# Second MoE of a fused attention and two-MoE kernel: fold the first weights of all eight experts while the tokens are sorted, fetch folded weights per tile, split the second weights by halves

## The reference

```python
x = attention(q, k, v)                    # 3072 tokens x 512
logits = x @ phi                          # first MoE: 8 experts x 4 slots = 32 slots
d = softmax(logits, axis=0); c = softmax(logits, axis=1)
slot_out[e] = relu((d.T @ x)[e] @ w1[e]) @ w2[e]
x = c @ slot_out                          # 3072 x 512, of rank 32
# second MoE, top-1
logits = x @ w_gate                       # 3072 x 8
idx = argmax(logits); gate_w = softmax(logits)[idx]
for e in range(8):                        # experts that have tokens
    h = relu(x[idx == e] @ w1[e])         # 512 -> 1024
    out[idx == e] = gate_w * (h @ w2[e])  # 1024 -> 512
```

## Time and profile before

| | |
|---|---|
| median of 3 runs | 518.71 us (517.88 to 519.81) |
| the profiled execution | 519.71 us, its span 518.0 us |
| mean granted TensorE clock | 0.913 of full |
| PE busy | 456.3 us (88%) |
| DVE, ACT, POOL busy | 246.5, 197.9, 202.5 us |
| moved by DMA | 89.79 MB |
| attention and first MoE | to about 272 us of the span |
| routing | about 272 to 307 us |
| second MoE's expert work | about 307 to 518 us |

### The profile page before, as it was taken

How to read it: one execution, slowest core, us unless ns; L and a number is a source line. 1 busy time by engine, 2 the same in 40 slices (tenths; PEclk the granted TensorE clock), 3 DMA queues, 4 the chain that set the end, 5 groups by cost and what they waited for, 6 DMA issues and landing times. The chain is left out here.

```text
span 518.0 us, 9323 instructions
## 1 busy us (share of the span) xinstructions
PE 456.3 (88%) x3119; PEld 377.8 (73%) x3120; DVE 246.5 (48%) x793; ACT 197.9 (38%) x399; POOL 202.5 (39%) x182
## 2 busy tenths in 40 slices
PE   7899999999999899989985055999999999999771
PEld 7699999999999877544455043888888887887451
DVE  5457777776777633641113947233332333332451
ACT  1568877877877444111000013122222122222420
POOL 2879888888886001010000001233333333333200
PEclk9879999999999989979985557999999999999976
DMA  6598898867661088499920357211111111111100
GB/s 232 211 411 331 331 381 323 340 232 262 233 237 59 4 310 341 140 387 384 407 103 1 140 189 273 82 51 38 43 51 51 51 51 51 51 51 51 44 2 5
DMA packets 27236, 89.79 MB, mean 173 GB/s; under 512 B 3344, under 2 KB 3344, under 8 KB 27200
## 3 DMA queue, kind: packets, MB, share of 16 engines
q1 hardware_dynamic: 23936, 79.70, 41.1%
q0 software_dynamic: 3264, 9.64, 5.3%
HBM read 81.46 MB, written 8.13 MB: 173 GB/s over the span
## 5 line engine op out<-in xcount | busy, mean ns | idle before, releaser
L435 ACT ACTIVATE Pb<-Pb,nm 128x256 f32<-128x256 f32 (+1 forms) x192 | 83.7, 484 | 35.4 <-DVE nm L536 35.4
L1466 DVE SCALAR_TENSOR_TENSOR hl<-Hq,hh 128x512 fp32r<-128x512 f32 x54 | 37.3, 691 | 123.5 <-ACT hh L1435 123.5
L382 PE MATMUL O<-V,PTs 128*128 128x65 f32 x704 | 91.7, 272 | 0.0
L382 PEld LDWEIGHTS O<-V,PTs 128*128 128x128 f32 x704 | 88.3, 195 | 1.0 <-issue 1.0
L536 DVE CUSTOM_DVE_ANT_0 Pb<-S,TA 128x256 f32<-128x256 f32 (+1 forms) x192 | 68.7, 396 | 37.2 <-PE S L355 35.2
L1410 PE MATMUL Yq<-w2h,hh 128*128 128x512 f32 x200 | 84.9, 425 | 0.3 <-DVE hl L1466 0.3
L1411 PE MATMUL Yq<-w2l,hh 128*128 128x512 f32 x200 | 79.6, 398 | 0.0
L1412 PE MATMUL Yq<-w2h,hl 128*128 128x512 f32 x200 | 79.4, 397 | 0.0
L1435 ACT ACTIVATE hh<-Hq 128x512 fp32r<-128x512 f32 x54 | 32.3, 598 | 115.9 <-PE Hq L1374 87.7
L313 POOL TENSOR_TENSOR kl<-k_raw,kh 128x1632 fp32r<-128x1632 f32 x15 | 55.2, 3679 | 9.9 <-ACT kh L445 9.7
L364 PE MATMUL PT<-ident,Pb 128*128 128x128 f32 x352 | 55.9, 278 | 0.9 <-ACT Pb L435 0.9
(11 more groups left out here) (222 smaller groups left out, 585.2 us busy)
## 6 DMA issues: line engine op xcount, KB each, us to landing
mem<-in_moe_w SPq DMA_DIRECT2D x14, 2048.0 KB, 11.4
k_raw<-in_k SPq DMA_DIRECT2D x16, 816.0 KB, 7.5
q_raw<-in_q SPq DMA_DIRECT2D x16, 768.0 KB, 5.6
ext<-in_moe_w SPq DMA_DIRECT2D x6, 2048.0 KB, 19.0
V<-in_v SPq DMA_DIRECT2D x16, 715.0 KB, 4.5
c_rows<-XL POOLq DMA_DIRECT2D x1, 1536.0 KB, 14.0
Cg<-c_rows,src POOLq DMA_INDIRECT x27, 2.5
out<-Ysb,dst POOLq DMA_INDIRECT x25
```

What stands on the lines that cost most here:

```text
L382: mm = pe.matmul(O[grp % 2][:, at:at + VC], PTs[:, par, (h * kbs + kb) * P:(h * kbs + kb + 1) * P], V[:, buf, h, vb, :], start=(n == 0), s ...
L435: nc.scalar.activation(Pb[:, par, h, 0:width(g)], Pb[:, par, h, 0:width(g)], ACT.Exp, bias=nm[:, par, h:h + 1], scale=-1.0).then_inc(exp_d ...
```

## The change

- `soft_moe` also transposes `Cn` to `CT` (in a free part of `mem`), on PE after the second expert's hidden products, and SP goes on after the 16 pieces with the first weights of the second MoE, experts 0 to 5, each into the slot named by `v1_slot` once that slot's piece is used.
- `routing` and `top1_moe` are one block. PE runs 16 *units* (8 experts x 2 halves) of the fold among the sorting's matmuls: two before the rank matmuls, ten before the 24 sorting matmuls, four after. In a unit, ACT does the copies, and the remainder is made on PE: a matmul with `-I` subtracts the rounded value in place, and ACT copies the result to the lower 64 rows. All folded weights stay in `Gall`. `C4` is ordered high, remainder, high, remainder to match.
- Per tile, ACT issues two DMAs that copy the half of a tile's expert from `Gall` to `Gst` inside the on-chip memory, the number of the expert being read from a table `te`.
- The second weights of the next expert are split chunk by chunk as each half of the last tile's products is done. An expert change has no fold.
- POOL gathers three tiles ahead, copies the source column before it waits for `cg_turned`, and the destination column before it waits for `y_scaled`. DVE does `low(u, 1)`, `low(u + 1, 0)` and then the scaling of tile u, which was behind both halves of `low(u + 1)` before.

The diff, cut to its core:

```diff
@@ build
+        v1_loaded = [sem(f"v1_loaded{e}") for e in range(NE)]
+def v1_slot(mem, e):
+    n = [MEMW, MEMW + 1, 0, 1, 2, 3, MEMW, MEMW + 1][e]
+    return mem[:, n, :]
@@ soft_moe, SP
             load_piece(sp, i, slot(i))
+        for e in range(XSLOTS - 1 + MEMW):
+            sp.wait_ge(piece_used, MEMW + EXT + e + 1)
+            load_v1(sp, e)
@@ soft_moe, PE
             if e + 1 < NE:
                 hidden(e + 1)
+            if e == 0:
+                pe.wait_ge(c_done, 1)
+                for g in range(TT // REP):
+                    mm = pe.transpose((Mp if g < 4 else SIg)[...], Cn[...], ident[:])
+                mm.then_inc(ct_turned, 1)
@@ top1_moe, SP
+        for e in range(2):
+            sp.wait_ge(gp_done, 2 * e + 2)
+            load_v1(sp, NE - 2 + e)
+        sp.wait_ge(gp_done, 6)
+        sp.wait_ge(rt_ready, 1)
+        load_v2(sp, entry(sp, 0, 0))
@@ top1_moe, POOL
+        for u in range(3):
+            gather(u, u)
+        with pool.Fori(0, total) as u:
+            gather(u + 3, u + 2 + (u + 2 <= total))
+            pool.wait_ge(row_free, u + 1)
+            nc.gpsimd.tensor_copy(dst1[:], dst_i[...]).then_inc(dst_copied, 1)
+            pool.wait_ge(dst_copied, u + 1)
+            pool.wait_ge(y_scaled, u + 3)
...
@@ top1_moe, PE
+        def products(n):
+            e, half = n // 2, n % 2
+            if half == 0:
+                pe.wait_ge(v1_loaded[e], 16)
+            if n >= 4:
+                pe.wait_ge(g_low, n - 3)
+            for c in range(DC):
+                mm = pe.matmul(Gp[c * SLOTS:(c + 1) * SLOTS, n % 4, :], STR[:, c, 0, :],
+                               v1_slot(mem, e)[:, at:at + 512], ...)
+        def joined(n):
+            pe.wait_ge(gp_out, n + 1)
+            pe.matmul(Gp[:, n % 4, :], Rsel[...], Gpart[:, n % 4, :], ...)
+        def remainder(n):
+            pe.wait_ge(g_high, n + 1)
+            pe.matmul(Gp[:, n % 4, :], nident[:], Gall[...], start=False, ...)
+        def units(which):
+            for n in which:
+                if n < UNITS:
+                    products(n)
+                if 1 <= n <= UNITS:
+                    joined(n - 1)
+                if n >= 2:
+                    remainder(n - 2)
@@ hidden(u, half)
+            pe.wait_ge(g_here[half], (u + 1) * 16)
@@ top1_moe, ACT
+        for n in range(UNITS + 2):
+            if n < UNITS:
+                parts_out(n)
...
+            if 1 <= n <= UNITS:
+                high(n - 1)
+            if n >= 2:
+                low(n - 2)
+        act.wait_ge(g_low, 2 * NE)
+        for half in range(2):
+            fetch(e0, half)
+        act.wait_ge(v2_loaded, 16)
+        act.wait_ge(sorted_done, 1)
+        for ch in range(W2CH):
+            nc.scalar.copy(w2h[:, chunk(ch)], raw[:, chunk(ch)]).then_inc(w2_high, 1)
...
+            with act.Fori(0, tiles) as j:
+                u = first + j
+                ahead = [expert(u + 1), expert(u + 2)]
+                relu(u, 1)
+                fetch(ahead[0], 1)
+                turned_out(u + 1)
+                relu(u + 1, 0)
+                fetch(ahead[1], 0)
+            act.wait_ge(v2_loaded, (rank + 1 + (rank + 1 < used)) * 16)
+            with act.Fori(0, chunks_after(rank, used)) as ch:
+                act.wait_ge(y_half, (first + tiles) * 2 + 1 + (ch >> 1))
+                nc.scalar.copy(w2h[:, chunk(ch)], raw[:, chunk(ch)]).then_inc(w2_high, 1)
@@ top1_moe, DVE
+            with dve.Fori(0, tiles) as j:
+                low(u, 1)
+                low(u + 1, 0)
+                with dve.If(u > 0):
+                    dve.wait_ge(stored, u * 16)
+                dve.sem_inc(row_free, 1)
+                dve.wait_ge(y_half, u * 2 + 4)
+                v.tensor_scalar(Ysb, Yq[...], gate_s[...], None, ALU.mult).then_inc(y_scaled, 1)
+            with dve.Fori(0, chunks_after(rank, used)) as ch:
+                dve.wait_ge(w2_high, rank * W2CH + W2CH + 1 + ch)
+                remainders(ch)
```

More of the change, by code:

```diff
@@ L719, in soft_moe @@
     st_out = sem("st_out")
+    ct_turned = sem("ct_turned")
+    ct_out = sem("ct_out")
     block = nc.Block()
@@ L1074, in _ @@
-        load_v(sp, e, True)
+        load_v2(sp, entry(sp, 0, 0))
+        used = count(sp)
+        with sp.If(used > 1):
+            with sp.Fori(1, used) as r:
+                e = entry(sp, r, 0)
+                sp.wait_ge(w2_low, r * W2CH)
+                sp.sem_inc(sp_passed, 1)
+                load_v2(sp, e)
     @block.gpsimd
@@ L1092, in _, with turn, hidden @@
+        def turn(u):
+            pe.wait_ge(gathered, u * 16 + 16)
+            pe.transpose(Cp[:, 0:P], Cg[:], ident[:]).then_inc(cg_turned, 1)
+        def hidden(u, half):
+            pe.wait_ge(g_here[half], (u + 1) * 16)
+            for fc in range(half * 4, half * 4 + 4):
+                mm = pe.matmul(Hq[half][:, (fc % 4) * P:(fc % 4 + 1) * P],
+                               Gst[:, fc * P:(fc + 1) * P], CgT[:], start=True, stop=True)
+            mm.then_inc(hid_done, 1)
         for c in range(DC):
-            mm = pe.matmul(Gp[:, 0:NE], STR[:, c].rearrange("p r s -> p (r s)"), wg_sb[:, c, :],
+            mm = pe.matmul(GWp, STR[:, c].rearrange("p r s -> p (r s)"), wg_sb[:, c, :],
@@ L1113, in _ @@
         mm.then_inc(sorted_done, 1)
+        units(range(2 * (NE - 2), UNITS + 2))
+        turn(0)
+        pe.wait_ge(cgt_out, 1)
+        for half in range(2):
+            hidden(0, half)
+        with pe.Fori(0, count(pe)) as rank:
+            tiles, first = entry(pe, rank, 1), entry(pe, rank, 2)
+            with pe.Fori(0, tiles) as j:
+                u = first + j
+                pe.wait_ge(y_scaled, u + 1)
+                Y = Yq[:, bass.ds(u % 2, 1), :].rearrange("p a d -> p (a d)")
+                for half in range(2):
+                    pe.wait_ge(w2_low, rank * W2CH + (half + 1) * W2CH // 2)
+                    pe.wait_ge(hid_low, u * 2 + (half + 1))
+                    for fc in range(half * 4, half * 4 + 4):
+                        cols = slice(fc * D, (fc + 1) * D)
+                        pe.matmul(Y, hh[:, fc, :], w2h[:, cols], start=(fc == 0), stop=False)
+                        pe.matmul(Y, hh[:, fc, :], w2l[:, cols], start=False, stop=False)
+                        mm = pe.matmul(Y, hl[:, fc, :], w2h[:, cols], start=False, stop=(fc == FC - 1))
+                        if fc == 1:
+                            turn(u + 1)
+                    mm.then_inc(y_half, 1)
+                    if half == 0:
+                        pe.wait_ge(cgt_out, u + 2)
+                    hidden(u + 1, half)
@@ L1124, in _ @@
+        total = all_tiles(act)
+        for half in range(2):
+            act.wait_ge(g_here[half], (total + 2 - half) * 16)
+        act.sem_inc(act_passed, 1)
     @block.vector
```

523 lines of the change are left out of this document (235 added, 288 removed).

## The result

The change made the kernel **slower**: median 523.92 us (519.62 to 527.85, 20 runs) against 520.83 us (515.42 to 524.47, 20 runs) of the kernel before, a ratio of 1.0067 with a 95% interval of 1.0043 to 1.0092. The forecast was 509 us, with a range of 500 to 518.

What follows compares the result with a forecast made beforehand. The prediction took PE to set the pace in the tiles, 6.69 us each. Its terms, 0 + 7.7 - 5.2 - 12.5 = -10.0 us, gave 509.7 from the profiled 519.71 and 508.7 from the median; it said 509, range 500 to 518.

Steps and rivals of the forecast that it cites:

- the fold: Between routing and first products: folding all eight experts, 2.1 us a unit, is on the path and adds 7.7 us.
- First MoE's part: First MoE's block: added transposes cancel and six early weight loads delay nothing; 0 us, bounds -1 to +1.5.
- Rivals 1, 2 and 5: Fold hidden, 501 us, chance 0.20; units at 2.6 us, 516, 0.13; half clock through the fold, 533, 0.04.
- The steady tiles: Tile loop: an earlier gather removes the transpose's stall, tiles go from 6.69 to 6.50 us; -5.2 us in total.
- rival 3: Steady tiles: the gather stall stays because POOL's order only moves it; 514 us, chance 0.10.
- The fetch: Per-tile copy of folded weights, 256 KB: lands in 3.1 us with 4.4 us left, so costs 0.
- Rival 4: Wait ahead of the hidden values: the fetch is late in every tile; 530 us at 5.3 us landing, chance 0.07.
- Expert change and end: From the end of tile 23 to the last scatter: 13.5 us against 25.97, so -12.5 us.
- Scaling to 0.85: At the expert change: DVE's scaling is done 0.85 us after tile 23's end, and PE starts tile 24 at 3.6.

Runs made afterwards that it cites:

- e7: Changed kernel with five early loads, second weights in four pieces, scatter before gather, no unneeded gather, first split on DVE during the fold: 510.25 us, ratio 0.9824.
- e3: Changed kernel with POOL's scatter of a tile put ahead of the gather for three tiles later: 524.10 us, ratio 1.0087.
- e1: Changed kernel with five early weight loads in the first MoE's block, the sixth at the start of the next block: 518.92 us, ratio 0.9994.
- e4: Kernel before the change, with only DVE's scaling moved between the two halves of the next remainder: 513.27 us, ratio 0.9885.
- e2: Changed kernel with the 2 MB load of the next expert's second weights cut into four pieces, one per tile: 518.49 us, ratio 0.9979.
- e5: e1's kernel with the next expert's second weights loaded in one piece only after tile 10 is scaled: 520.26 us, one run.
- e8: e7's kernel with idle PE products, 16 while the first fetch lands and 10 at each expert change: 506.21 us, ratio 0.9739.

## Why the prediction was wrong

**The sign.** I gave slower 0.11. The sum had the right mechanisms for the fold and most of the end, and lacked two losses of 5 to 6 us each; a smaller gain at the end took 3 more. With the losses repaired most of the forecast's 10 us are there (e7 is 1.76%, 9.2 us, under before), though e7 has the gains of e3 and of the earlier split as well.

**First MoE's part, priced 0.** The step that failed is "The six early loads of first weights use a queue that is then idle and stand behind all pieces on SP, so they delay none." They delay no piece. They delay the block's end, since the last one's issue takes 10.38 us and all engines wait for SP there. Nor was the queue idle: the first of the six is issued at 247.7, in slice 20, where the kernel before still moves 407 GB/s. I took an issue at 0.4 us, from the earlier trace rows, four loads with at most one other outstanding. The trace of the kernel before held the other number, and my sum passed over it. The answer on its line of the pieces, L93, with issues in ns, least, median and most:

```profile
L93 SPq DMA_DIRECT2D ext<-in_moe_w x6: 379/1831/8707, 182.2 to 242.2; - x6
```

The cost was 5.6 us in the profile; e1 takes back all of that, and 3.8 (by the ratios) to 5.0 us of the time.

**The fold, priced +7.7.** Right: +8.2, with a longer unit and an earlier start. Timeline of the kernel after, PE, one unit:

```profile
287.57 1.07 PE L1254 MATMUL Gp<-mem,STR 128*32 128x512 f32 x8
288.57 1.12 PE L1262 MATMUL Gp<-mem,Rsel 128*128 128x512 f32 x2
289.13 0.80 PE L1269 MATMUL Gp<-Gall,nident 128*128 128x512 f32 x1
289.86 1.06 PE L1254 MATMUL Gp<-mem,STR 128*32 128x512 f32 x8
```

A unit takes 2.29 us of PE, products 1.00, join 0.56 and remainder 0.73, where I had 2.1 (0.96, 0.87 and 0.23): the join was sized too long and the remainder, a third of the unit, far too short. These errors cancel in part, and the gate logits end 5.3 us after the block's start instead of 6.6, a gain that I had booked in the first MoE's part, so the close hit on this item is partly luck. Four of my dates, counted from PE's first instruction of the block: sorting matmuls at 33.3, found 33.6; fold drained 47.1, found 48.3; fetches issued 48.6, found 50.3; first products 57.0, found 57.6. The order of the steps, sorting matmuls, drain, fetches, split, held. Rivals 1, 2 and 5 (hidden; 2.6 us a unit; half clock, 3.8 us) fall with it.

**The steady tiles, priced -5.2.** The gather's stall did go: 6.49 us a tile, PE never idle, 4.0 us over tiles 3 to 22 and 5.4 over tiles 2 to 23; rival 3 falls. The scatter's wait of 3.1 us is hidden, as I had it. e4 shows that the order on DVE alone does this. All of it was given back at the first two tiles: 12.2 and 8.7 us, where the kernel before took 8.3 and 6.5.

**The fetch, priced 0.** In 23 of 24 tiles right: none is waited for, and e7's land in 2.2 to 2.6 us, like the gather and unlike the 3.1 I took. The estimate of 4.0 us was worked out from figures that the Trainium skill, "DMA: Bandwidth & Descriptors", "Bandwidth", gives for loads from HBM issued by GpSimd; for this copy, issued by ACT inside the on-chip memory with the engines else little used, it is too long. Rival 4 had the right mechanism and the wrong place. The step that failed is its "from the second tile on no weights are loaded", by which I set it aside: I never put the next expert's 2 MB load, which the change issues in tile 0, on the same clock as the fetches of tile 0. A landing of 8.8 us, once, costs the 3.5 of the wait and some 2 of half clock behind it. That this load is the cause is shown by e2 (in pieces: gone) and e5 (moved: the stall moves with it). The packets in the trace show the delay in two parts. The load's packets run from 333.9 on, and ACT's queue moves none of the fetch issued at 334.47 until 338.45, 4.0 us after its issue, where the fetch before it (issued 330.25) began to move after 1.2 us. Then that queue, on which a further fetch stands by now (issued 337.06), shares the engines with the load for nearly 5 us. The gather of e5 is held up in the same way: its first packet comes 5.3 us after its issue.

The Trainium skill, "DMA: Bandwidth & Descriptors", "Queues, rings and completion order", says that each DMA engine takes turns between queues packet by packet. By such turns a fetch of 256 KB would get something near a third to a half of the engines and land in about 4 us (an estimate; a third of 400 GB/s moves 256 KB in 2 us, where alone it takes 0.65). The 8.8 us here are longer, and the measurement decides; why the fetch moves nothing for its first 4 us was not tried.

**Expert change and end, priced -12.5.** -9.6. The step is "Scaling to 0.85": it had forgotten that the scaling waits for the scatter, which I had myself put behind the gather. It ran at 1.6 to 2.4 us, PE started at 5.0 instead of 3.6, and the scatter of tile 23 landed in 3.7 us instead of 3.1. My cover for this wait was that of a steady tile; at the expert change DVE's next work is on the path. e3 gives 13.4, where I had forecast 13.5, and shows at once what else POOL's order holds; e8, at full clock throughout, gives 11.9, and my bound for that was 12.

**Range.** It left out that two losses can add, and one of the two, the block's end, stood in no rival. Each loss alone would have given about 514, within the range.

## What to carry to other kernels

The price of a DMA issue is not fixed, it was 0.37 to 10.38 us on one line of this kernel: before a load is put at the end of a block, look up the longest issue of that queue, not the shortest. When small latency-bound copies are made per tile, write every large load of the same stretch next to them in order of time, and cut it into pieces that fit the copies' slack. And try a change's smallest part alone: e4, one operation moved, gains 1.2% where the whole change lost 0.7 and its repaired form e7 gains 1.8.

## What the hardware showed that I had not expected

- An SP issue of a 2 MB load took 0.37 to 10.38 us (L98 in the kernel after); in e2, which has the sixth load there too, the longest was 10.38 again, in e1 5.13.
- A small transfer issued 0.1 to 1.6 us behind a 2 MB load on another queue landed after 8.1 us (gather, e5) and 8.8 (fetch, after), against 2.5 and 2.3 alone.
- In both cases the small transfer's queue moved nothing for 4.0 and 5.3 us after the issue, while the load's packets ran.
- Idle matmuls pay: 36 short products without use, 16 ahead of the first tile and 10 at the end of each expert, took 4.0 us off the median (e8 against e7), most of it at the expert change. The granted clock is lost in a wait of 2.5 us (0.58 in the 4 us behind it in e5), so that this wait cost about 1.6 times its length; behind the 1.2 us wait of e1 it was 1.00.
- Five register reads in a row on ACT ahead of a relu (the number of experts, an expert's tiles and first tile, the experts of two tiles) leave it 3.6 us without work; five at the spacing of the earlier trace rows, 0.63, are 3.2 of them. Timeline of e7, ACT:

```profile
326.74 0.60 ACT L1395 ACTIVATE hh<-Gp 128x512 fp32r<-128x512 f32 x1 [3.58 <-issue]
```
